# Attention with routing and MoE on one core: similarities and turnings back laid one by one between transposes

## What is computed

```python
def _attn_ref(q, k, v, centroids):            # (2, 8, 768, 64); 16 centroids for each of 8 heads
    ...
    q_assign = np.argmax(np.einsum('bhsd,hcd->bhsc', q_n, c_n), axis=-1)
    k_assign = np.argmax(np.einsum('bhsd,hcd->bhsc', k_n, c_n), axis=-1)
    mask = q_assign[:, :, :, None] == k_assign[:, :, None, :]
    scores = scale * np.matmul(q, k.transpose(0, 1, 3, 2))
    scores = np.where(mask, scores, -1000000000.0)
    ...
    return np.matmul(softmax(scores), v)
# reference(): x = attention as (1536, 512)
#   x = top-1 mixture of 8 experts, 512 -> 1024 -> 512, relu
#   out = ((x @ w_a) * (x @ w_b)) @ w_out, 512 -> 1536 -> 512
```

## Time and profile before

| what | value |
|---|---|
| time, median of 3 runs | 809.46 us (809.43 to 809.65) |
| the profiled execution | 809.58 us, its span 807.8 us |
| PE busy | 797.6 us (99%), 4412 matmuls |
| PE weight loads (PEld) busy | 678.3 us (84%) |
| DVE busy | 459.1 us (57%) |
| ACT busy | 359.0 us (44%) |
| POOL busy | 365.2 us (45%) |
| granted clock of PE | full, mean 1.000 |

### The profile page before, as it was taken

How to read it: one execution, slowest core, us unless ns; L and a number is a source line. 1 busy time by engine, 2 the same in 40 slices (tenths; PEclk the granted TensorE clock), 3 DMA queues, 4 the chain that set the end, 5 groups by cost and what they waited for, 6 DMA issues and landing times.

```text
span 807.8 us, 13176 instructions
## 1 busy us (share of the span) xinstructions
PE 797.6 (99%) x4412; PEld 678.3 (84%) x4413; DVE 459.1 (57%) x716; ACT 359.0 (44%) x740; POOL 365.2 (45%) x311
## 2 busy tenths in 40 slices
PE   8999999999999999999999999999999999999997
PEld 5899999999998688888888888888888888888886
DVE  5987988988997989999867004531211112121211
ACT  7877867877786443443434444111212112121112
POOL 6798898888982354464454634000311002010001
PEclk9999999999999999999999999999999999999999
DMA  7463363363242487888677313300101000010001
GB/s 202 115 190 95 105 185 94 102 187 95 63 125 84 152 255 201 250 251 253 220 212 235 113 41 99 123 1 14 27 14 53 1 14 13 1 53 0 1 1 52
DMA packets 48665, 86.62 MB, mean 107 GB/s; under 512 B 17856, under 2 KB 19904, under 8 KB 48624
## 3 DMA queue, kind: packets, MB, share of 16 engines
q1 hardware_dynamic: 41888, 69.36, 29.9%
q0 software_dynamic: 3856, 11.33, 4.9%
q10 hardware_dynamic: 2880, 5.39, 1.8%
HBM read 73.29 MB, written 11.30 MB: 105 GB/s over the span
## 4 chain that ended last, share of the span: by engine, by line
PE 77%; issue 16%; DVE 2%; DMA 2%; POOL 1%; ACT 1%; SPq 0%; POOLq 0%; DVEq 0%
PE bank L1729 9%; PE bank L1659 9%; PE bank L1463 7%; PE bank L1626 7%; PE bank L1628 7%; PE bank L1627 7%; PE bank L1666 4%; PE bank L1733 4%; PE bank L1432 4%; PE bank L1477 4%; PE bank L1453 4%; PE bank L1479 3%; PE bank L1501 2%; PE bank L1391 2%; PE bank L1673 2%
## 5 line engine op out<-in xcount | busy, mean ns | idle before, releaser
L1355 DVE TENSOR_TENSOR ab_raw<-bank,a_sb 128x512 f32<-128x512 f32 x35 | 24.2, 692 | 183.9 <-PE bank L1628 183.9
L409 DVE CAST w_split<-stage 128x1024 fp32r<-128x1024 f32 x68 | 70.0, 1029 | 68.2 <-PE bank L1666 52.7
L1128 DVE TENSOR_REDUCE neg_max<-bank 128x1 f32<-128x768 f32 x96 | 91.6, 955 | 23.4 <-PE bank L1453 22.5
L846 ACT ACTIVATE pT_hi<-bank 128x384 fp32r<-128x384 f32 x192 | 83.9, 490 | 43.0 <-PE bank L1463 42.4
L413 DVE TENSOR_TENSOR w_split<-stage,w_split 128x1024 fp32r<-128x1024 f32 x72 | 99.3, 1382 | 2.4
L1096 DVE TENSOR_TENSOR pT_lo<-bank,pT_hi 128x384 fp32r<-128x384 f32 x192 | 97.5, 550 | 2.2 <-ACT pT_hi L846 1.7
L717 POOL TENSOR_TENSOR hT_lo<-hT_raw,hT_hi 128x512 fp32r<-128x512 f32 x38 | 54.6, 1437 | 78.0 <-ACT hT_raw L921 77.9
L866 ACT ACTIVATE probs<-bank,neg_max 128x768 f32<-128x768 f32 x96 | 87.1, 907 | 3.4 <-DVE neg_max L1128 3.2
L1729 PE MATMUL bank<-w_split,hT_hi 128*128 (+1 forms) x304 | 79.5, 404 | 0.0
L981 ACT ACTIVATE a_sb<-bank 128x512 f32<-128x512 f32 x35 | 20.9, 597 | 131.9 <-PE bank L1628 131.9
L1463 PE MATMUL bank<-ident,probs 128*128 128x128 f32 x576 | 78.9, 273 | 0.1
(11 more groups left out here) (269 smaller groups left out, 1735.9 us busy)
## 6 DMA issues: line engine op xcount, KB each, us to landing
stage<-w SPq DMA_DIRECT2D x64, 512.0 KB, 4.5
q_raw<-qT SPq DMA_DIRECT2D x32, 192.0 KB, 3.7
k_raw<-kT SPq DMA_DIRECT2D x32, 192.0 KB, 4.0
sorted_y<-y_sb ACTq DMA_DIRECT2D x19, 257.0 KB, 4.7
q_pair<-qT SPq DMA_DIRECT2D x8, 384.0 KB, 4.7
v_raw<-v_keys SPq DMA_DIRECT2D x16, 192.0 KB, 4.1
stage<-w_a SPq DMA_DIRECT2D x6, 512.0 KB, 4.6
stage<-w_b SPq DMA_DIRECT2D x6, 512.0 KB, 4.9
```

The source lines that it names most:

```text
L1128: dve.tensor_reduce(neg_max[:, qt % 2:qt % 2 + 1], scores[qt % 2][:, 0:S], AX_X, ALU.max, negate=True).then_inc(s_max, 1)
```

## The change

It moves instructions on PE and DVE and adds none. `turn_back_tile` and `similarity` are single products, and `transpose_probs` and `probs_v` lay them ahead of their own.
- Pairs of the loop: similarities 0 to 2 stand ahead of the transposes of the second half in step 0, 3 to 5 ahead of the low products of step 0, 6 to 8 ahead of the transposes of the first half in step 1, 9 to 11 ahead of those of the second half in step 2. In pair 0 the first three stay a block, the other nine stand ahead of the second half's transposes in steps 2 to 4.
- The three turnings back of steps 1 and 4 stand ahead of the three transposes of the second half of the same step. Those of the last head stay as they were.
- DVE does `scale_x` between the pT_lo of the first and of the second half.

```diff
--- before.py
+++ after.py
@@ -1088,9 +1088,9 @@
                                       first_idx[:, :].unsqueeze(2).to_broadcast([P, 4 * QT, C]),
                                       ALU.is_equal).then_inc(s_hot, 1)
 
-            def evacuate(n, qt, pT_ps=pT_ps):
+            def evacuate(n, qt, pT_ps=pT_ps, parts=range(2)):
                 half, j = qt // GT, qt % GT
-                for part in range(2):
+                for part in parts:
                     dst = (slice(None), half, slice(part * GT, (part + 1) * GT), slice(j * P, (j + 1) * P))
                     dve.wait_ge(s_ph, 2 * n + part + 1)
                     dve.tensor_tensor(pT_lo[dst], pT_ps[part].rearrange("p (k q) -> p k q", q=P),
@@ -1127,14 +1127,16 @@
                     dve.wait_ge(s_S, n + 1)
                     dve.tensor_reduce(neg_max[:, qt % 2:qt % 2 + 1], scores[qt % 2][:, 0:S], AX_X, ALU.max,
                                       negate=True).then_inc(s_max, 1)
-                    if before or qt >= 2:
+                    if before and qt % GT == 1:
+                        evacuate(n - 2, (qt - 2) % QT, parts=(0,))
+                        scale_x(g - 1, pp - 1 + slot, 1 - slot, qt // GT)
+                        evacuate(n - 2, (qt - 2) % QT, parts=(1,))
+                    elif before or qt >= 2:
                         evacuate(n - 2, (qt - 2) % QT)
                     if before and qt == 0:
                         row_norm(g - 1, 1 - slot)
                     for step in steps.get((slot, qt), ()) if more else ():
                         assign(pp + 1, step)
-                    if before and qt % GT == 1:
-                        scale_x(g - 1, pp - 1 + slot, 1 - slot, qt // GT)
                     if static(pp) and pp == PAIRS - 1:
                         early_routing(slot * QT + qt)
 
@@ -1390,16 +1392,15 @@
                 raw = (q_pair, k_pair)[t % 2]
                 return pe.matmul(out, raw[:, t // 2 * P:(t // 2 + 1) * P], cT, start=True, stop=True)
 
-            def similarities(pp, tiles):
-                if tiles[0] == 0:
+            def similarity(pp, t):
+                if t == 0:
                     if static(pp) and pp == 1:
                         pe.wait_ge(s_cTs, 6)
                     pe.wait_ge(s_pair, 32 * (pp + 1))
                     pe.wait_ge(s_hotr, pp)
-                for t in tiles:
-                    last = sim_rows(pp, t, sims[:, t * 2 * C:(t + 1) * 2 * C])
-                if tiles[-1] == 2 * QT - 1:
-                    last.then_inc(s_sims, 1)
+                done = sim_rows(pp, t, sims[:, t * 2 * C:(t + 1) * 2 * C])
+                if t == 2 * QT - 1:
+                    done.then_inc(s_sims, 1)
 
             def first_similarities(half):
                 for t in range(QT):
@@ -1453,18 +1454,22 @@
                     last = pe.matmul(ps[:, lo:hi], q_lm[0:D + C, slot, at], k_hm[0:D + C, slot, lo:hi], start=False, stop=True)
                 last.then_inc(s_S, 1)
 
-            def transpose_probs(n, slot, pT_ps=pT_ps):
+            def transpose_probs(n, slot, pT_ps=pT_ps, pp=None, first_sim=(None, None), back=None):
                 pe.wait_ge(s_exp, n + 1)
                 for part, done in ((0, s_TA), (1, s_TB)):
                     if not static(n) or 1 <= n < G * QT - 1:
                         pe.wait_ge(s_pl, 2 * n - 1 + part)
                     for j in range(QT // 2):
                         kt = part * (QT // 2) + j
+                        if first_sim[part] is not None:
+                            similarity(pp, first_sim[part] + j)
+                        if back is not None and part == 1:
+                            turn_back_tile(*back, j)
                         last = pe.transpose(pT_ps[part][:, j * P:(j + 1) * P], probs[:, slot, kt * P:(kt + 1) * P], ident[:, :])
                     last.then_inc(done, 1)
 
 
-            def probs_v(g, slot, half, key_tiles, oT_ps=oT_ps):
+            def probs_v(g, slot, half, key_tiles, oT_ps=oT_ps, pp=None, first_sim=None):
                 if key_tiles[0] == 0:
                     pe.wait_ge(s_pl, 2 * (g * QT + (half + 1) * GT))
                     pe.wait_ge(s_vs, g + 1)
@@ -1474,6 +1479,8 @@
                     hi_lo = v_split[:, slot, kt].rearrange("p two d -> p (two d)")
                     if kt == 0:
                         pe.matmul(oT_ps, hi_lo, pT_hi[:, half, kt], start=True, stop=False)
+                    if first_sim is not None:
+                        similarity(pp, first_sim + kt - key_tiles[0])
                     pe.matmul(oT_ps[0:D], v_split[:, slot, kt, 0], pT_lo[:, half, kt], start=False, stop=False)
                     if kt > 0:
                         last = pe.matmul(oT_ps, hi_lo, pT_hi[:, half, kt], start=False, stop=(kt == QT - 1))
@@ -1492,14 +1499,19 @@
                 pe.matmul(last_oT_ps, v_split[:, slot, QT - 1].rearrange("p two d -> p (two d)"), pT_hi[:, 1, QT - 1],
                           start=False, stop=True).then_inc(s_pv, 1)
 
+            def turn_back_tile(g, half, j, x_ps=x_ps, o_T=o_T):
+                if j == 0:
+                    pe.wait_ge(s_oT, 2 * g + half + 1)
+                    if static(g) and g == 0 and half == 0:
+                        pe.wait_ge(s_bw, 4)
+                w = back_w[:, bass.ds(g, 1), :].rearrange("p g w -> p (g w)")
+                done = pe.matmul(x_ps[:, j, :], o_T[:, j * P:(j + 1) * P], w, start=True, stop=True)
+                if j == GT - 1:
+                    done.then_inc(s_back, 1)
+
             def turn_back(g, half, x_ps=x_ps, o_T=o_T):
-                pe.wait_ge(s_oT, 2 * g + half + 1)
-                if static(g) and g == 0 and half == 0:
-                    pe.wait_ge(s_bw, 4)
-                w = back_w[:, bass.ds(g, 1), :].rearrange("p g w -> p (g w)")
                 for j in range(GT):
-                    last = pe.matmul(x_ps[:, j, :], o_T[:, j * P:(j + 1) * P], w, start=True, stop=True)
-                last.then_inc(s_back, 1)
+                    turn_back_tile(g, half, j, x_ps, o_T)
 
 
             def head(pp, slot):
@@ -1507,24 +1519,24 @@
                 more = not static(pp) or pp + 1 < PAIRS
                 before = not static(g) or g >= 1
                 first = static(pp) and pp == 0
-                sim_tiles = {qt: range(3 * qt - 3, 3 * qt) for qt in range(1, 5)} if first else {0: range(6), 1: range(6, 12)}
+                sim = more and slot == 0
+                sims_by_transposes = ({2: (None, 3), 3: (None, 6), 4: (None, 9)} if first else
+                                      {0: (None, 0), 1: (6, None), 2: (None, 9)}) if sim else {}
                 for qt in range(QT):
                     n = g * QT + qt
                     score(pp, g, n, slot, qt)
                     if before or qt >= 2:
-                        transpose_probs(n - 2, qt % 2)
+                        transpose_probs(n - 2, qt % 2, pp=pp + 1, first_sim=sims_by_transposes.get(qt, (None, None)),
+                                        back=(g - 1, qt // GT) if before and qt % GT == 1 else None)
                     if first and (slot, qt) == (0, 1):
                         spin(2)
-                    if more and slot == 0 and qt in sim_tiles:
-                        similarities(pp + 1, sim_tiles[qt])
-                    if first and (slot, qt) == (0, 1):
+                        for t in range(3):
+                            similarity(pp + 1, t)
                         spin(2)
-                    if before and qt % GT == 1:
-                        turn_back(g - 1, qt // GT)
                     if before and qt == 2:
                         probs_v(g - 1, 1 - slot, 1, range(GT))
                     if before and qt % GT == 0:
-                        probs_v(g - 1, 1 - slot, qt // GT, range(GT, QT))
+                        probs_v(g - 1, 1 - slot, qt // GT, range(GT, QT), pp=pp + 1, first_sim=3 if sim and qt == 0 else None)
                     if qt == QT - 1:
                         probs_v(g, slot, 0, range(GT))
                     if more and slot == 1 and qt == (3 if first else 1):
```

## The result

The change runs in 814.43 us (median of 4, 814.3 to 814.91) beside 809.44 us for the kernel before on the same chip (4 runs, 809.32 to 809.65): +5.0 us, ratio 1.0062, 95% interval 1.0045 to 1.008. The forecast was 811.9, slower by 2.4 us, its range 803 to 815. The likeliest case's own range ended at 814.4, so it is the fourth rival's 813 to 814.5, which the range took in, that holds this time.

A forecast was written before the change was run, and what follows sets the result against it. PE was taken as the bound, busy 797.6 of 807.8 us. Terms -4.3 - 4.5 - 2.6 + 9.5 + 0.3 + 4.0 = +2.4 us gave 811.9 us against the median, range 803 to 815.

The forecast's parts named there:

- The likeliest case: The forecast's summed terms, slower by 2.4 us at 811.9 us; chance 0.60, own range 809.4 to 814.4.
- the fourth rival: DVE becomes the bound: its new waits for pT_hi add 0.2 to 0.4 us per loop pair; 813 to 814.5 us; chance 0.05.
- What short matmuls cost: On PE beside transposes: similarity 0.167 us, not 0.22 (81, -4.3 us); turning back 0.174 each (30 blocks, -4.5 us).
- The new wait: PE waits 0.35 us for DVE's second low before the next step's fourth transpose, 27 times: +9.5 us.
- the chain: From the second half's last transpose through ACT and DVE to PE's fourth transpose of the next step: 1.38 us.
- The +0.3 behind step 7: In six loop pairs, six one-hot transposes behind step 7 leave 0.05 us of wait each time: +0.3 us.
- o_T: Earlier turnings back wait on PE for ACT's copy: 0.10, 0.21, 0.27 us in steps 4, 7, 10; +4.0 us in all.
- The scaling: DVE's scaling between its two lows readies x_head about 1 us earlier, ending PE's wait in step 5: -2.6 us.
- The sum by places: Check by place: loop pair +0.17 us (+1.0 for six), last pair +1.0, first pair +0.55 for similarities, -0.25 for the rest.
- no load hidden: Rival: a similarity costs 0.22 us anywhere and turnings back 0.67 a block on PE; 820.7 us; chance 0.07.
- the gain without the wait: Rival: PE's fourth transpose of the next step finds its bank free; 802.1 us; chance 0.18.
- half the wait: Rival: ACT and DVE hand back the bank in 1.2 us and o_T costs half; 805 us; chance 0.10.

The follow-up runs named there:

- the repeated transposes: The change, with the first half's three transposes done twice in the 24 steps behind a turning back without one-hot transposes: 814.89 us, ratio 1.0065.

## Why the prediction was right, and half in size

- **What short matmuls cost**: right. A turning back between transposes 0.175 to 0.18 (0.174 forecast), a similarity 0.175 (0.167). Measured over a pair the similarity gained 0.044, not 0.053: 81 of them 3.5 us, not 4.3. The transpose's short load (141 ns beside 192, both of 128 columns) is borne out. The Trainium skill's rule (TensorE: Matmul & The Clock Gate, section LDWEIGHTS) that the load goes by columns alone does not hold for it: by that rule the similarities alone would have gained nothing, and they gained 2.3 us.
- **The new wait**: right in kind, place, number and size. 27 waits of 0.36 to 0.41 against 27 of 0.35; the repeated transposes show that it is a wait for the chain. What was left out is the uncovered load of a similarity behind it, about 0.1 us in step 2 and in the first pair. The +0.3 behind step 7 did not come: step 8 takes 2.49 us before and 2.48 after.
- **o_T**: 0.10 and 0.27 us in steps 4 and 10 were right; step 7 took 0.31, not 0.21. But the term is not additive: with the copy made earlier only 1.4 us came back, of the 4.0, and other waits grew.
- **The scaling**: right for the change, wrong as a price of its own. Within the change the waits for x_head went, and the scaling filled DVE's wait for pT_hi, as forecast. Against its old place it is worth 0.39 us per loop pair there, where I had 0.31. But my price came from x_head alone. Alone DVE's order cost 3.0 us, because then DVE has no wait for the scaling to fill; and beside the turnings back in the halves, taking the wait for x_head away by another place left the change 2.2 to 2.5 us slower, so what the place between the lows saves is DVE's time.
- **The sum by places**: the last pair was right (0.93 against 1.0). The loop pair was off by 0.25, which makes 1.5 us of the 2.6 missed in all: similarities 0.1, the uncovered load 0.06, o_T in step 7 most of the rest. The first pair was off by 1.0: +1.30 instead of +0.3. Of this 0.24 lies ahead of all that moved, and is no effect of the change. Steps 2 to 5, with the similarities and their waits, came to +0.75 where I had 0.55, and of the -0.25 that I had for the rest +0.3 came. My own terms give about 0 there, not -0.25 (two new waits 0.7 and o_T 0.3, less 0.7 for x_head and 0.3 for two blocks). And DVE runs late there, exp and the copy o_T with it: the turning back of its step 10 starts 1.50 us into the step. What this lateness costs by itself was not tried.
- **The rivals**: no load hidden is excluded by the 0.175, the gain without the wait and half the wait by 27 waits of 0.36 to 0.41. DVE as the bound had 0.05, and the time fell into its 813 to 814.5, but not by its mechanism: its sign was DVE without idle time in steps 2 to 8, and DVE idles 0.42 us in step 2 and 0.20 in step 3. From step 4 to 8 it hardly idles, but so it was before. How near this bound lies, the scaling behind the lows shows: the maximum 0.29 us later cost 0.33 us per pair.
- **Luck**: that the range held the time is in part luck. The mechanism was the likeliest case's, its terms too small in sum, and the measured time lies 0.03 us outside that case's own range; 0.24 us of the profile's growth had nothing to do with the change.

## What to carry to other kernels

Matmuls with few columns gained here (0.044 us each) when they stood beside ones whose loads are short, but the instruction behind which they are put becomes later: before moving one ahead of a result that other engines take over, add up the way from that result back to the next use of its bank, and put in front only what the work behind it leaves room for. A block of small work behind the last transpose looked like waste and was the cover of a 1.4 us round through two engines. And the place of a small operation on the second engine has no price of its own: between the same two operations it cost 3.0 us with one order of PE and, against the same old place, won some 2.3 us in the six loop pairs with another (an estimate, from 0.39 per pair).

## What the runs showed of the hardware

- The load of a 128-column transpose of float32 takes 141 ns, like that of 64 columns (135), a plain one of 128 columns 192. Behind a similarity or turning back the transpose's load shows 0.19 to 0.23 us. Between transposes a two-load matmul of 32 or of 72 columns costs about the same, 0.175 to 0.18 us, which fits that the loads set it.
- From the end of DVE's second low to the waiting transpose are about 0.12 us (181.98 to 182.10), 0.05 of them until its load starts (182.03). A similarity or turning back that has waited takes longer to the transpose behind it than one that has not, 0.25 us for 0.14 and 0.26 for 0.17.
